# Dealing the model rows as 4p+d, with results turned by VectorE in 32x32 blocks and stored in runs of 128 values

## The reference

```python
# 1. windowed and dilated attention, per head
attn = softmax(where(mask, q @ k.T / 8, -1e9)) @ v
x = attn.transpose(0, 2, 1, 3).reshape(B, S, 512)
# 2. feed-forward with a shifted mix
x_prev = shift of x by one token
xk = mu_k * x + (1 - mu_k) * x_prev;  xr = mu_r * x + (1 - mu_r) * x_prev
k = relu(xk @ w_k);  v = (k * k) @ w_v;  r = sigmoid(xr @ w_r)     # w_k 512x1024, w_v 1024x512, w_r 512x512
x = r * v
# 3. mixer
h = relu(x.T @ w_tok1) @ w_tok2          # over tokens, 576 -> 256 -> 576
u = x + h.T
out = u + relu(u @ w_ch1) @ w_ch2        # over channels, 512 -> 1536 -> 512
```

## Time and profile before

| What | Value |
|---|---|
| Median of 3 runs | 779.47 us (777.72 to 779.48) |
| The profiled execution | 778.34 us, its span 776.5 us |
| Mean granted clock of TensorE in the profile | 0.977 |
| PE busy | 737.7 us, 95% of the span |
| DVE, ACT, POOL busy | 357.8, 259.4, 220.2 us |

### The profile page before, as it was taken

One profiled execution on the slowest core, in us unless ns is written; L12 is line 12 of the kernel. 1 busy time (PEld: TensorE's weight loads), 2 busy tenths in 40 slices (PEclk: granted clock), 3 DMA queues, 4 the chain that ended last, 5 costly groups with the idle time before them and its releaser, 6 DMA issues.

```text
span 776.5 us, 15690 instructions
## 1 busy us (share of the span) xinstructions
PE 737.7 (95%) x6630; PEld 714.6 (92%) x6630; DVE 357.8 (46%) x594; ACT 259.4 (33%) x645; POOL 220.2 (28%) x237
## 2 busy tenths in 40 slices
PE   6678999999999999999999999999999999999997
PEld 5567999899898989989999999999999999999997
DVE  5556956757475765758672122511225121341211
ACT  3555363443535354354442112311124111241111
POOL 4348563554655364554308100000000000000000
PEclk8569999999999999999999999999999999999999
DMA  9902231221211302020270100110002100010001
GB/s 216 271 1 49 61 73 38 58 52 36 59 46 32 68 18 60 19 62 1 104 283 2 62 1 1 62 62 1 2 1 89 34 1 1 1 62 2 1 1 61
DMA packets 67940, 39.80 MB, mean 51 GB/s; under 512 B 55263, under 2 KB 59167, under 8 KB 67871
## 3 DMA queue, kind: packets, MB, share of 16 engines
q1 hardware_dynamic: 64127, 33.69, 16.6%
q0 software_dynamic: 1088, 4.72, 1.8%
q10 hardware_dynamic: 2656, 0.40, 0.3%
HBM read 29.36 MB, written 4.72 MB: 44 GB/s over the span
## 4 chain that ended last, share of the span: by engine, by line
PE 82%; POOL 7%; DVE 4%; issue 3%; ACT 3%; DMA 1%; SPq 0%; ACTq 0%; DVEq 0%; POOLq 0%
PE bank L681 14%; PE bank L682 12%; PE bank L683 12%; PE tq L681 5%; PE tq L683 5%; PE tq L682 5%; PE bank L1108 3%; PE s L1108 3%; PE bank L1107 3%; PE bank L1106 3%; PE s L1106 3%; PE s L1107 3%; PE bank L602 3%; PE bank L574 2%; PE tq L437 2%
## 5 line engine op out<-in xcount | busy, mean ns | idle before, releaser
L681 PE MATMUL bank<-xk_hi,WK_hi 128*128 128x288 f32 x256 | 81.0, 316 | 17.8 <-DVE kr L734 11.3
L681 PE MATMUL bank<-k_hi,WV_hi 128*128 128x288 f32 x256 | 78.3, 306 | 0.0
L682 PE MATMUL bank<-xk_hi,WK_lo 128*128 128x288 f32 x256 | 76.5, 299 | 0.0
L683 PE MATMUL bank<-xk_lo,WK_hi 128*128 128x288 f32 x256 | 76.2, 298 | 0.0
L682 PE MATMUL bank<-k_hi,WV_lo 128*128 128x288 f32 x256 | 75.6, 295 | 0.0
L683 PE MATMUL bank<-k_lo,WV_hi 128*128 128x288 f32 x256 | 75.4, 294 | 0.0
L1082 DVE SCALAR_TENSOR_TENSOR h_lo<-tq,h_hi 128x288 fp32r<-128x288 f32 x48 | 22.0, 457 | 115.9 <-ACT h_hi L1078 115.9
L1082 DVE SCALAR_TENSOR_TENSOR h_lo<-bank,h_hi 128x288 fp32r<-128x288 f32 x48 | 22.0, 457 | 115.5 <-ACT h_hi L1078 115.5
L749 POOL TENSOR_TENSOR k_lo<-kr,k_hi 128x288 fp32r<-128x288 f32 x64 | 53.5, 837 | 72.1 <-ACT k_hi L745 71.9
L681 PEld LDWEIGHTS bank<-xk_hi,WK_hi 128*128 128x128 f32 x256 | 48.9, 191 | 21.7 <-DVE kr L734 13.1
L782 DVE RECIPROCAL rg<-rg 128x288 f32<-128x288 f32 x32 | 62.5, 1953 | 1.1
(11 more groups left out here) (149 smaller groups left out, 2121.5 us busy)
## 6 DMA issues: line engine op xcount, KB each, us to landing
C_raw<-in_moe_w_ch SPq DMA_DIRECT2D x6, 1024.0 KB, 11.7
xcur<-X POOLq DMA_DIRECT2D x4, 1152.0 KB, 5.7
qraw<-in_q SPq DMA_DIRECT2D x20, 192.0 KB, 3.4
kraw<-in_k SPq DMA_DIRECT2D x20, 192.0 KB, 4.0
out_x<-ost SPq DMA_DIRECT2D x16, 240.0 KB, 2.6
vt<-in_v SPq DMA_DIRECT2D x40, 80.0 KB, 2.5
vt<-in_v SPq DMA_DIRECT2D x7, 320.0 KB, 3.4
WK_raw<-in_moe_w_k SPq DMA_DIRECT2D x4, 512.0 KB, 5.4
```

Of the source, the lines that this page charges most:

```text
L681: e.matmul(out_ap, wh, xh, start=start and i == 0, stop=False)
L682: e.matmul(out_ap, wl, xh, start=False, stop=False)
L683: last = e.matmul(out_ap, wh, xl, start=False, stop=stop and i == len(kts) - 1)
```

## The change

Model row 4p+d now lies in tile d at partition p, from the outputs of the gate and the down product on (`WR`, `WV`), through `X`, `U`, `C1`'s rows and the outputs of `C2`. The columns of w_r, w_v and w_ch2 are dealt in the split: raw data is loaded as before with rows contiguous, and ACT, DVE and POOL read it with a step of four values (`by_tile`). For that the raw data can't lie under `lo` any more: w_r's is loaded into the part of `X` that belongs to sequence 1, w_v's into the parts of sequences 3 and 2, whose first content (the raw q and k, and v, of attention steps 2 and 3) must have been read; w_ch2's raw tiles lie one tile behind `C2_lo`, so each tile is split by itself in order. w_ch1 is loaded with rows 4p..4p+3 on a partition.

The output path changes too. `out_transpose` is gone. DVE turns `U` in 32x32 blocks (`out_blocks`) into `blocks`, where each partition then holds, for 9 tokens, 128 values that are contiguous in the output; the store is 4 transfers per half, each of 32 partitions x 9 runs of 128 values. `finish` now goes tile by tile, each with its own wait. The bank order `ORDER` loses its five `ot` entries.

```diff
+        def raw_tile(b, t):
+            c0 = b * XB + t * XC + 1
+            return X[:, c0:c0 + DM]
+        def by_tile(ap):
+            return ap.rearrange("p (q d) -> p d q", d=DT)
+        def load_wv(half):
+            def sync(e):
+                if half == 0:
+                    e.wait_ge(Z.tk_done, 4)
+                else:
+                    e.wait_ge(Z.o_done, 4)
+                e.dma_start(raw_tiles(3 - half), kview(w_v)[:, DT * half:DT * (half + 1), :]).then_inc(wv_in[half], 16)
...
         def split_wr(i):
-            hi, lo, raw = parts(WR, P, SPLIT * i, SPLIT)
+            hi, lo = [tiles(t, DT) for t in parts(WR, P, DM * i, DM)]
+            raw = by_tile(raw_tile(1, i))
...
         def split_wv(i):
-            hi, lo, raw = parts(WV, P, SPLIT * i, SPLIT)
+            hi, lo = [tiles(t, DT) for t in parts(WV, P, DM * i, DM)]
+            raw = by_tile(raw_tile(3 - i // DT, i % DT))
...
-        pieces2 += [[c2_block(t, 0) for t in C2] + [c2_in[0], 16]]
+        pieces2 += [[*c2_tile(f), c2_in[0], 16] for f in range(4)]
...
-                     load_weights1(w_r, WR, 0, 4, Z.wr_in),
-                     load_weights1(w_v, WV, 0, 4, wv_in[0]), load_weights1(w_v, WV, 4, 4, wv_in[1]), load_qk(2)]
+                     load_wr(), load_qk(2), load_wv(0), load_wv(1)]
...
-                [("x", i) for i in range(NTT)] + [("t1", i) for i in range(2)] + [("ot", i) for i in range(NTT)]
+                [("x", i) for i in range(NTT)] + [("t1", i) for i in range(2)]
...
-        def out_transpose(b, tt):
...
+        def out_blocks(b, h, d):
+            def vector(e):
+                e.wait_ge(Z.fin_done, 8 * b + 4 * h + d + 1)
+                if d == 0:
+                    wait(e, out_done[h], 64 * b)
+                e.transpose(blocks[h][:, :].rearrange("p (c q d) -> p d c q", d=DT, q=32)[:, d],
+                            U[:, S * d + HALF * h:S * d + HALF * (h + 1)]).then_inc(Z.ob_done, 1)
+            return dict(vector=vector)
+        def store(b, h):
+            def one(e, g):
+                e.wait_ge(Z.ob_done, 8 * b + 4 * h + 4)
+                e.dma_start(out[b, HALF * h:HALF * (h + 1), P * g:P * (g + 1)].rearrange("(c i) n -> i c n", i=32),
+                            blocks[h][32 * g:32 * (g + 1), :].rearrange("p (c n) -> p c n", n=P)).then_inc(out_done[h], 16)
...
-            return steps + ups + [out_transpose(b, tt) for tt in range(NTT)]
+            return steps + [store(b, 0), store(b, 1)] + ups
```

More of the change, by code:

```diff
@@ L105, in build @@
         kr = at("kr", [P, NKR * HALF], F32, o); o += 4 * NKR * HALF
[L106 removed]
+        WV_offset = o
+        WV, o = split("WV", [P, FT1 * DM], o)
         k2_offset = o
@@ L136, in build @@
         h2, o = split("h2", [P, NH2 * HALF], o)
-        ost = [at(f"ost{i}", [P, DM], F32, 4 * DM * i) for i in range(4)] + [at("ost4", [P, DM], F32, o)]
-        assert NTT == 5 and 4 * DM <= XB
-        o += 4 * DM
+        blocks = [at(f"blocks{h}", [P, DT * HALF], F32, 4 * DT * HALF * h) for h in range(2)]
         xcur = at("xcur", [P, DT * S], F32, o); o += 4 * DT * S
@@ L313, in gpsimd @@
                 e.wait_ge(Z.ul_done, 8)
-                e.tensor_copy(hi, raw).then_inc(Z.c2w_done, 1)
-                e.wait_ge(Z.c2w_done, 2 * j - 1)
-                e.tensor_tensor(lo, raw, hi.bitcast(F32), ALU.subtract).then_inc(Z.c2w_done, 1)
+                if j == 1:
+                    e.wait_ge(Z.w_lo2, N_2)
+                for f in range(4 * j, 4 * j + 4):
+                    hi, lo, raw = c2_tile(f)
+                    n = 2 * (f - 4)
+                    wait(e, Z.c2w_done, n)
+                    e.tensor_copy(hi, raw).then_inc(Z.c2w_done, 1)
+                    e.wait_ge(Z.c2w_done, n + 1)
+                    e.tensor_tensor(lo, raw, hi.bitcast(F32), ALU.subtract).then_inc(Z.c2w_done, 1)
             return dict(gpsimd=gpsimd)
@@ L936, in work_free @@
                 b, before = b - 1, before + TB
-            if kind == "ot" and i < 4 and b == B - 1:
-                return e.wait_ge(Z.h2l_done, 2 * FT2 * (b + 1))
             k, n = ORDER[before]
             s, per, ahead = READ[k]
-            wait(e, s, per * (b + ahead) + n + 1 + (NTT if k == "ot" else 0))
+            wait(e, s, per * (b + ahead) + n + 1)
         def rows_of(tt):
@@ L1117, in finish @@
             return dict(vector=vector)
-        def out_transpose(b, tt):
[L1120 to L1129, removed]
-            def scalar(e):
[L1132 to L1143, removed]
@@ new lines, in build, with sync @@
+        out_done = (Z.out_done0, Z.out_done1)
+        def out_blocks(b, h, d):
[11 more added lines that the diff above has]
+                            blocks[h][32 * g:32 * (g + 1), :].rearrange("p (c n) -> p c n", n=P)).then_inc(out_done[h], 16)
+            def sync(e):
+                for g in range(2 if (b, h) == (B - 1, 1) else 4):
+                    one(e, g)
+            def scalar(e):
+                for g in range(2, 4):
+                    one(e, g)
+            return dict(sync=sync, scalar=scalar) if (b, h) == (B - 1, 1) else dict(sync=sync)
```

98 lines of the change are left out of this document (57 added, 41 removed).

## The result

The changed kernel takes 781.45 us (median of 13 runs) beside 778.98 us of the kernel before in the same series: +2.5 us. That is slower by a little more than the 0.3% that can be told from no change. The forecast was 780.1 us, +1.8 us. The profiled execution took 782.26 us, its span 780.5 us, 4.0 us more than the span of before.

A forecast was written before the change was run, and what follows sets the result against it. PE is busy 95% of the span, but from 52 to 80 us the chain runs over POOL. Early +3.2, phases +1.3, boundaries -2.5, tail -0.2 on the profiled 778.34 us gave 780.1 us, range 774.8 to 783.

The forecast's parts named there:

- The boundaries: Between sequences, `token_down` starts without PE's transposes, saving what stands behind the `h_lo` wait: 0.84 us, three times, -2.5 us.
- The tail: Behind the last matmul: adds tile by tile, block transposes at 0.63 us, four stores; -0.2 us, between -1.8 and +1.3.
- The change of phases: DVE's four stepped pieces instead of one delay the first piece's `h_lo`, which PE awaits: +1.3 us, zero if reads are free.
- The early term: Between 52 and 80 us, stepped splits lengthen the chain: two ACT, one DVE at 0.54, four POOL at 0.4; +3.2 us.
- Free reads: Rival: only stepped writes pay, or slack hides the splits; early and phase costs zero, 775.6 us; chance 0.28.
- Dear transposes or stores: Rival: block transposes at 1.95 us each lengthen the tail and cancel the boundary gain; 788 us; chance 0.07.
- POOL pays more: Rival: stepped reads cost POOL 0.8 us per split, early cost 4.8, 781.7 us; far side of the 0.65 case.
- main case: Stepped reads pay in the splits: 780.1 us, own range 777.5 to 782.5; chance 0.65.
- The signs: Profile after: splits 1.1 to 1.3 us on ACT and DVE, POOL 1.6 or more; transposes near 83, `token_down` 4.5 later.

The follow-up runs named there:

- oldout: Changed kernel with the output path of before put back (PE transposes of U, ACT copies, five stores), splits still stepped; 783.99 us, ratio 1.0074.
- warm: Changed kernel with 8, 3 and 3 more identity matmuls, results unused, ahead of units 5, 6 and 7 of the feed-forward; 781.38 us, ratio 1.0023.
- plain_c2: Changed kernel with w_ch2's tiles read plainly in their splits, w_r and w_v still stepped; 780.73 us, ratio 1.0034.
- dve_plain: `warm` with only DVE's lo pieces of w_r and w_v read plainly, ACT and POOL still stepped; 779.19 us, ratio 1.0009.
- pool_plain: `warm` with only POOL's lo pieces of w_v read plainly, ACT and DVE still stepped; 779.77 us, ratio 1.0010.
- reorder: Changed kernel with next sequence's transposes a step earlier, `token_up` ahead of the last `channel_down`, last half's block transposes delayed; 777.04 us, ratio 0.9975.

## Why the prediction came out as it did

The time lies inside the stated range (774.8 to 783), 1.4 us over the forecast, and slower by a little over 0.3%, a class to which I gave 0.32 and not the 0.42 of the likeliest.

**The boundaries, -2.5 us: right.** R goes from 361.1 to 358.5, `oldout` gives it back. The gap was forecast at 1.4 us and is 1.46. The gain was the part behind the wait, not the transposes' 2.4 us each.

**The tail, -0.2 us: right**, in part by luck, as two errors offset each other. 7.2 us before and 6.9 us after, from the end of the last matmul. The block transpose takes 0.67 us (0.63 forecast); DVE ends 2.5 us behind the last matmul (2.9 forecast), and the last transfer is issued somewhat later than thought.

**The change of phases, +1.3 us: right in sum, by luck.** M grew by 1.26 us, and the five DVE pieces by 2.3 us, as forecast. But two errors of opposite sign cancel: the step costs DVE 0.38 us a piece, not 0.54, and waiting piece by piece 0.8 us, not 0.2.

**The early term, +3.2 us: too small.** This is the step that failed, in size. From `kr` on the profile of the changed kernel has 5.0 us more than that of before; with the clock held (`warm`) it is 4.8 us, and `oldout` and `plain_c2` have 4.7. The chain of before shows where, beside that of `warm` (two of the pieces that grew most; start, duration, what):

```profile
58.93 0.77 POOL k_lo L749
...
60.91 1.44 POOL sm L521
```
```profile
59.79 1.49 POOL k_lo L793
...
62.26 1.95 POOL sm L565
```

My three sums were 1.1 us for two ACT pieces, 0.5 for one DVE piece, 1.6 for four POOL pieces. On the chains the two ACT pieces grow by 1.1 us, the DVE piece by 0.4, and the four POOL pieces from 1.23 to 1.25 us each to 1.49 to 1.52, so by 1.05 us in all: 2.5 us for the splits, less than forecast. The other 2.3 us are POOL's remaining instructions on the chain, `k_lo` and the softmax's, which read what they read before and for which I had nothing. `dve_plain` shows most of their cause: it takes 2.2 us off, where DVE's own piece is worth 0.4. The other DVE pieces are beside the chain, but POOL's instructions that begin next to them become longer by about as much as they do, and POOL is the chain. The prices can't simply be added: `dve_plain` takes off 2.2 us, `pool_plain` 2.1 and ACT's pieces have grown by 1.1, which is more than 4.8, so what one engine's step costs depends on the others'. No run reads plainly on ACT alone.

**The sum.** 1.8 forecast, 1.6 for the early term (4.8 for 3.2), 0.2 for the fall of the clock, 0.2 for the part of E ahead of `kr` (11.1 for 10.9) and 0.4 for the first 41 us (41.73 for 41.34, the same code for PE) make 4.2; the boundaries and the tail gave back 0.2 more than forecast, which leaves the 4.0 us of the spans. On the medians the difference is smaller, 2.5 for 1.8 us, since the profiled execution of before lay 0.6 us under its median and that of the changed kernel 0.8 us over its own.

**The rivals.** Free reads: refuted by every stepped row. Dear transposes or stores: refuted by 0.67 us and by a tail that got shorter. That "nearly all rows of 288 values lie between 0.3 and 0.5 us" was too strong, though: of DVE's 416 such instructions in before, 96 take 0.83 or 1.95 us on average. POOL pays more: the time came close to that rival's 781.7 us, and it was nearer to the truth than the main case. Its early term was 4.8 us, as measured, with 0.8 us for each POOL split because POOL shares the time with DVE. Its place was wrong: the splits themselves pay 0.26 us each, and the instructions around them the rest, which makes 3.3 us on POOL for its 3.2.

**The signs.** ACT's 1.13 us and DVE's 1.07 and more are as foretold; POOL's 1.54 is a little under "1.6 or more". PE reached the transposes at 85.42, not near 83. The first `token_down` came 6.0 us later, not 4.5; and 4.5 was a slip, since by the prediction's own terms the boundary gives back 0.8 us just ahead of it, which leaves 3.7. The main case's own range was narrow as well: POOL free or at twice its price together with the tail's bounds give 776.9 to 783.2, not 777.5 to 782.5.

## What to carry to other kernels

When an instruction beside the chain gets longer, ask what it shares with the engine that is the chain, not only whether it lies on it. Before paying in compute for a better memory layout, try the worse layout in the transfer that it was meant for: here runs of 128 bytes cost nothing, since the stores lie under matmuls (R is 358.5 us with either). And when PE waits for a stretch, look for other work that can stand in that place: moving splits into idle time and one step of matmuls across a boundary was worth more than the whole change.

## What the runs showed of the hardware

For 512 fp32 values on 128 partitions, a read with a step of 16 bytes in place of a plain one takes ACT from 0.62 to 1.13 us, DVE (two operands, one of them stepped) from 0.69 to 1.07, and POOL (the same) from between 1.08 and 1.29 to 1.54. The Trainium skill (GPSIMD Engine Reference, Performance pitfalls for Q7 kernels) has 50% more for such reads on POOL; these rows have 19 to 43%. A block transpose of 128x288 fp32 takes 0.67 us into a stepped destination and 0.46 into a plain one.

The granted clock of PE fell to its lower level (0.50) behind a wait of 2.21 us, and what that costs depends on where it falls: 0.2 to 0.3 us in the changed kernel's profile, 1.8 us in that of `reorder`, where the slow matmuls lay on the chain. These prices come from one profile each. What the record gives ahead of the first fall is not PE's pace: with 1.00 on record (`reorder`) and with 0.50 (changed kernel) a matmul of 288 columns took 0.24 us up to some 52.4 us. So a high mean in an execution without a profile (before: 7 of 27) doesn't say that PE was faster. When PE takes up 0.13 us differs between executions, from 50.2 to 53.1 us in these profiles, and moves what follows by up to 1 us; why is open.
